# Three edits to a fused recurrent attention, low-rank mixing and gated FFN kernel: the order of the first loads, the slots of three mixing tiles, the order of the attention output products

## The reference: a recurrent state, then two dense layers

```
f = sigmoid(f_logit)
for t in tokens:   state = f[t, :, None] * state + outer(k[t], v[t]);   y[t] = q[t] @ state
x = y as (4, 768, 384)
u = x + (low-rank mixing over tokens: U is 768x32, V is 32x768)
x2 = u + relu(u @ w_ch1) @ w_ch2                       # 384 -> 1536 -> 384
h = relu(x2 @ w_in)                                    # 384 -> 1024
out = (h * sigmoid(conv3 over tokens of h)) @ w_out    # 1024 -> 384
```

## The kernel before, in words

| (par, ch) | quarter in kind 0 | quarter in kind 1 |
|---|---|---|
| (0, 0) | A: rows 0, columns 0 | A |
| (0, 1) | B: rows 0, columns 1 | C |
| (1, 0) | C: rows 1, columns 1 | B |
| (1, 1) | D: rows 1, columns 0 | D |

## Time and profile before

### The profile page before, as it was taken

How to read it: one execution, slowest core, us unless ns; L and a number is a source line. 1 busy time by engine, 2 the same in 40 slices (tenths; PEclk the granted TensorE clock), 3 DMA queues, 4 the chain that set the end, 5 groups by cost and what they waited for, 6 DMA issues and landing times.

```text
span 713.4 us, 22514 instructions
## 1 busy us (share of the span) xinstructions
PE 684.9 (96%) x10076; PEld 648.7 (91%) x10076; DVE 438.8 (62%) x744; ACT 248.8 (35%) x508; POOL 266.1 (37%) x243
## 2 busy tenths in 40 slices
PE   2888999999999999999999999999999999999997
PEld 1788799999999999999999899999999989999997
DVE  6886675674786764364597855365498651122875
ACT  1034534251355412223245432213145541121553
POOL 4872574463542333152263315143263220030432
PEclk9999999999999999999999999999999999999999
DMA  9331444432002111201201110200000100000000
GB/s 207 94 93 37 113 135 118 118 90 62 8 18 74 35 34 25 68 4 28 64 2 56 46 57 3 68 24 25 24 2 2 35 34 1 0 1 1 1 34 33
DMA packets 22719, 33.46 MB, mean 47 GB/s; under 512 B 3584, under 2 KB 15616, under 8 KB 22624
## 3 DMA queue, kind: packets, MB, share of 16 engines
q1 hardware_dynamic: 21616, 30.27, 15.4%
q10 hardware_dynamic: 1008, 1.77, 1.1%
HBM read 27.31 MB, written 4.72 MB: 45 GB/s over the span
## 4 chain that ended last, share of the span: by engine, by line
PE 91%; POOL 2%; DVE 2%; issue 2%; ACT 1%; DMA 1%; ACTq 0%; POOLq 0%; DVEq 0%
PE acc L751 8%; PE att L614 7%; PE hb L732 7%; PE acc L752 7%; PE acc L756 7%; PE hb L733 7%; PE hb L734 7%; PE acc L790 5%; PE hb L771 5%; PE hb L773 5%; PE hb L772 5%; PE acc L791 5%; PE acc L795 5%; PE att L660 3%; PE att L636 1%
## 5 line engine op out<-in xcount | busy, mean ns | idle before, releaser
L1138 DVE SCALAR_TENSOR_TENSOR r_lo<-hb,r_hi 128x386 fp32r<-128x386 f32 (+1 forms) x96 | 53.5, 557 | 179.1 <-ACT r_hi L914 179.1
L914 ACT ACTIVATE r_hi<-hb 128x386 fp32r<-128x386 f32 (+1 forms) x96 | 47.2, 491 | 248.8 <-PE hb L734 248.8
L1227 POOL TENSOR_TENSOR k_t<-k_t,blocks 112x512 f32<-112x512 f32 x60 | 81.2, 1356 | 135.0 <-PE att L614 127.2
L1266 POOL TENSOR_TENSOR r_lo<-conv,r_hi 128x384 fp32r<-128x384 f32 x64 | 63.3, 989 | 141.6 <-ACT r_hi L929 141.6
L751 PE MATMUL acc<-r_hi,w_ch_hi 128*128 128x386 f32 (+1 forms) x288 | 103.1, 358 | 0.0
L732 PE MATMUL hb<-u_hi,w_ch_hi 128*128 128x386 f32 (+1 forms) x288 | 98.1, 341 | 1.2 <-POOL w_ch_lo L1239 0.7
L733 PE MATMUL hb<-u_hi,w_ch_lo 128*128 128x386 f32 (+1 forms) x288 | 97.5, 339 | 0.0
L752 PE MATMUL acc<-r_hi,w_ch_lo 128*128 128x386 f32 (+1 forms) x288 | 97.3, 338 | 0.0
L734 PE MATMUL hb<-u_lo,w_ch_hi 128*128 128x386 f32 (+1 forms) x288 | 96.9, 336 | 0.0
L1168 DVE SCALAR_TENSOR_TENSOR conv<-hb,convw,conv 128x384 f32<-128x384 f32 x128 | 79.1, 618 | 4.5
L614 PEld LDWEIGHTS att<-q_t,k_t 48*64 48x64 f32 (+3 forms) x3840 | 59.3, 134 | 19.0 <-issue 13.2
(11 more groups left out here) (147 smaller groups left out, 1258.0 us busy)
## 6 DMA issues: line engine op xcount, KB each, us to landing
v_p<-in_vn_dram SPq DMA_DIRECT2D x12, 384.0 KB, 3.7
out_dram<-ostage SPq DMA_DIRECT2D x24, 192.0 KB, 2.1
q_t<-in_qT_dram SPq DMA_DIRECT2D x21, 192.0 KB, 3.5
k_t<-in_kT_dram SPq DMA_DIRECT2D x21, 192.0 KB, 3.4
gates<-in_fT_dram SPq DMA_DIRECT2D x21, 192.0 KB, 3.6
ostage<-in_w_ch_dram SPq DMA_DIRECT2D x14, 192.0 KB, 2.6
conv<-in_w_ch_dram SPq DMA_DIRECT2D x10, 192.0 KB, 3.0
ostage<-in_w_out_dram SPq DMA_DIRECT2D x5, 192.0 KB, 2.4
```

## The change

In words: (1) Loads of duos 0 to 2 go in the order gates, q, k on both queues; mask and identity are issued behind duo 0's loads. (2) GpSimd clears gates ahead of k, and takes over two of the three score buffers after that. (3) VectorE prepares identity and masks after gating q of duo 0, no longer ahead of the selves. (4) For duo 0 alone VectorE gates the even k itself, ahead of the even q, with a semaphore of its own (`k_first_ready`); GpSimd makes the gate-pair products of duo 0 as soon as the sigmoid is done. (5) Mixing tiles 3, 4 and 5 follow slots 0, 1 and 2. (6) The 64 output products of a duo are issued in another order, with the wait on `carried` behind 32 of them.

```diff
             if s < 2 * N1:
                 order.append(("first1", b, s))
-                if s < 2:
-                    order += [("mix", b, CT + i) for i in ([0], [1, 2])[s]]
+                if s < CT:
+                    order.append(("mix", b, CT + s))
...
-            consts()
             for task in ORDER:
...
+                    load_f(n)
                     load_q(n)
                     load_k(n)
-                    load_f(n)
+                    if n == 0:
+                        consts()
...
-                    pe.wait_ge(k_ready, gated(n, max(st - 1, 0)))
+                    k_gated(pe, n, max(st - 1, 0))
...
+                    for u in range(2):
+                        for r in range(PAIRS):
+                            add(0, u, r, 0, 0)
+                            add(0, u, r, 0, 1)
+                            mm = add(0, u, r, 1, 0)
+                    mm.then_inc(carried, 1)
+                    for r in range(PAIRS):
+                        add(0, 0, r, 1, 1)
+                        add(1, 0, r, 0, 0)
+                    pe.wait_ge(carried, outputs(n))
+                    for u in range(2):
+                        for r in range(PAIRS):
+                            add(1, u, r, 0, 1)
+                            add(1, u, r, 1, 0)
+                            add(u, 1 - u, r, 1, 1)
+                            mm = add(1, 1, r, u, u)
                     mm.then_inc(y_done, 1)
...
-            for i in range(3):
-                nc.vector.memset(scores[i][:], 0.0).then_inc(cleared_s, 1)
+            nc.vector.memset(scores[0][:], 0.0).then_inc(cleared_q, 1)
...
                     dve.wait_ge(gates_ready, n + 1)
                     dve.wait_ge(selves_ready, selves(n))
+                    if n == 0:
+                        nc.vector.tensor_tensor(even_k, even_k, split_blocks(gates[i][0:PR, :], 1)[:, :, 1, 0],
+                                                ALU.mult).then_inc(k_first_ready, 1)
                     nc.vector.tensor_tensor(even, even, split_blocks(gates[i][0:PR, :], 1)[:, :, 0, 0],
                                             ALU.mult).then_inc(q_ready, 1)
+                    if n == 0:
+                        constants()
...
             for i in range(3):
+                nc.gpsimd.memset(gates[i][32:64, :], 0.0).then_inc(cleared_k, 1)
                 nc.gpsimd.memset(k_t[i][32:64, :], 0.0).then_inc(cleared_k, 1)
-                nc.gpsimd.memset(gates[i][32:64, :], 0.0).then_inc(cleared_k, 1)
             pool.wait_ge(cleared_k, 6)
+            for i in range(1, 3):
+                nc.gpsimd.memset(scores[i][:], 0.0).then_inc(cleared_s, 1)
...
-                if st == 0:
+                if (n, st) == (0, 0):
+                    pool.wait_ge(gates_ready, 1)
+                elif st == 0:
```

More of the change, by code:

```diff
@@ L178 @@
 LAST_AT = numbered(lambda t: t[0] == "att" and t[2] == LEVELS - 1)
[L179 removed]
+GATED_AT = numbered(lambda t: t[0] == "att" and t[2] < LEVELS and t[2] != 0 and t[1:] != (0, EVEN))
 PAIRED_AT = numbered(lambda t: t[0] == "att" and t[2] in (EVEN, 1))
@@ L438, in products_made, with k_gated @@
                 engine.wait_ge(merged_ready, merged(n, st - 1))
+        def k_gated(engine, n, st):
+            if st == 0 and n == 0:
+                engine.wait_ge(k_first_ready, 1)
+            else:
+                engine.wait_ge(k_ready, gated(n, st))
         def weights_split(engine, n):
@@ L643, in attention @@
                     begun = set()
[L644 to L663, removed]
-                        if kind == 0:
-                            mm.then_inc(carried, 1)
-                            pe.wait_ge(carried, outputs(n))
@@ new lines, in add @@
+                    def add(kind, u, r, par, ch):
+                        cc, g, o = 2 * u + ch, u * PAIRS + r, C * (par ^ ch)
+                        gg = par * 2 * PAIRS + g
+                        if kind == 0 and j == 0 and cc == 0:
+                            return None
+                        if kind == 0:
+                            rows, first = slice(C * par, C * par + D), at(u, r, ch)
+                            lhsT = q[rows, first:first + C]
+                            rhs = state[rows, (4 * j + cc) % STATES, r, :]
+                        else:
+                            rows = slice(C * ch, C * ch + C)
+                            lhsT = scores[i][rows, gg * C:(gg + 1) * C]
+                            rhs = v_p[i][rows, 2 * g + par, :]
+                        start = (par, ch) not in begun
+                        begun.add((par, ch))
+                        return pe.matmul(banks[o:o + C, par, g * D:(g + 1) * D], lhsT, rhs, start=start,
+                                         stop=(kind == 1), skip_group_check=True)
@@ L823, in load @@
                     act.wait_ge(q_ready, scaled(0, EVEN))
+                act.wait_ge(cleared_k, 2 * n + 1)
+                act.dma_start(gates[n][odd, :].rearrange("d (u t) -> d u t", u=2),
+                              fT[0, 2 * n:2 * n + 2, 1].rearrange("u d t -> d u t")).then_inc(loaded_f[n], 16)
                 act.wait_ge(cleared_q, n + 1)
@@ L991, in _, with constants @@
                     nc.vector.memset(part[:, :, col:col + PAD].bitcast(F32), 0.0).then_inc(padded, 1)
[L992 to L1002, removed]
+            def constants():
+                dve.wait_ge(loaded_masks, 32)
+                nc.vector.tensor_copy(ident_r[:], x[:, 1, 0:P]).then_inc(padded, 1)
+                nc.vector.tensor_copy(masks[:].rearrange("p l t -> p (l t)"), x[:, 0, 0:LEVELS * 32]).then_inc(masks_ready, 1)
+                pair, odd = x[:, 0, 0:32], x[:, 0, 256:288]
+                units = x[:, 1, 0:P].rearrange("p (h n two) -> p h n two", h=2, two=2)
+                first = first_mask[:].rearrange("p (n two) -> p n two", two=2)
+                nc.vector.tensor_copy(first[:, :, 0], pair).then_inc(masks_ready, 1)
+                nc.vector.tensor_tensor(odd, units[:, 0, :, 1], units[:, 1, :, 1], ALU.add).then_inc(masks_ready, 1)
+                dve.wait_ge(masks_ready, 3)
+                nc.vector.tensor_tensor(first[:, :, 1], odd, pair, ALU.add).then_inc(masks_ready, 1)
             def take_scores(n, st):
@@ L1221, in attention @@
                     pool.wait_ge(level_done, levels(n, st))
-                    pool.wait_ge(k_ready, gated(n, st - 1))
+                    k_gated(pool, n, st - 1)
                     products_made(pool, n, st)
```

19 lines of the change are left out of this document (10 added, 9 removed).

## The result

The changed kernel has a median of 716.88 us (17 runs, 715.34 to 718.53), the kernel before 715.43 us in the same comparison (17 runs). The ratio is 1.0023, 95% interval 1.0013 to 1.0033: slower by 1.6 us (0.9 to 2.4). Forecast were 718.6 us and slower; the range, 715.2 to 721.6, holds it, but the likeliest case's size, +3.5, is more than twice the measured one. The profiled execution of after took 717.44 us, its span 715.6, 2.2 more than before.

The account below looks back on a forecast made before the run. TensorE, busy 96% of the span, was taken to bound the kernel. Terms -1.9 - 1.4 + 4.1 + 2.7 = +3.5 us on the profiled 715.21 gave 718.7, forecast as 718.6 us; 8-in-10 range 715.2 to 721.6.

Parts of the forecast that it names:

- start: Loads and gating of duo 0: level 0 starts near 11.35 instead of 13.21, -1.9 us (ends -2.4 and -1.2).
- mixing slots: First-FFN groups behind tile 5, batches 1 to 3: three waits on VectorE go, -1.4 us (ends -1.6 and 0).
- products, duos 3 to 11: Dense output products: quarter D ends last, 2.56 us instead of 2.10, nine times +0.46, +4.1 us (ends +3.6 and +5.8).
- products, duos 0 to 2: Slower output products at 0.106 us a round: 0.9 us each, all in the chain, +2.7 us (ends +1.5 and +3.3).
- the prediction's own borders: Whole kernel: faster below 713.0 us (0.14), slower above 717.2 (0.72), the same between (0.14); 0.3% is 2.1 us.
- rival b: Output products: each starts only after all ahead in the program; 48 rounds, 2.73 us, total 721.0 us; chance 0.06.
- The 23 loads: Duo 9's output products: 23 loads started after 0.47 us, in the ninth round; strict order gives at most 20.
- the cover of duo 1: Duo 1's loads: last may land at 14.7, needed at 15.2; if late, takes back at most some 0.5 us.
- the prediction's own signs of being wrong: Output group under 2.1 us, time below 715, or duo 1's selves waiting for k would show the forecast wrong.
- I carry the whole gain forward: From level 0 on each step is released by the one before, so the start's whole -1.9 us was kept.
- The prediction's 1.62 / 15: Duos 0 to 2: (1.84 - 0.22) / 15, given as 0.106 us a round of output products.
- rival (d): Duos 0 to 2: cost hidden behind ScalarE's copies and state updates, 58 to 76 us; 715.9 us, no change; chance 0.07.

Follow-up runs that it names:

- start alone: The kernel before with parts 1 to 4 of the change only (loads, clearings, constants, k of duo 0 on VectorE): 715.12 us, ratio 0.9989.
- constants first: The kernel before with the change's start, but the DMAs of masks and identity issued ahead of duo 0's gates, as before: 712.89 us, ratio 0.9947.
- 32 rounds behind the wait: The kernel before with the change's product order, but the four middle D products also behind the wait: 729.34 us, ratio 1.0189.
- balanced order alone: The kernel before with all kind 0 products, eight of kind 1 in A and D, the wait, then B and C: 714.06 us, ratio 0.9977.
- mixing slots with the balanced order: The kernel before with the change's mixing slots and the product order of balanced order alone: 712.85 us, ratio 0.9947.
- all three parts: The changed kernel with the masks' and identity's DMAs first and the product order of balanced order alone: 710.24 us over 4 runs, ratio 0.9904.

## Why the prediction was right and where it was wrong

| term | forecast | measured |
|---|---|---|
| start | -1.9 (-2.4 to -1.2) | -0.8 (-1.6 to +0.1), alone; 0.3 of it at the end of the span |
| mixing slots | -1.4 | -1.33 (three of 0.44 to 0.45) |
| products, duos 3 to 11 | +4.1 | +4.05 (nine of 0.45) |
| products, duos 0 to 2 | +2.7 | -0.4 (-1.2 to +0.4), alone |
| sum | +3.5 | +1.5; the change itself +1.6 |

The direction rests on the dense products, and they were right. The size is out by two misses of opposite sign: the start gave 1.1 us less than forecast, and duos 0 to 2 cost 3.1 us less. That they cancel in part is luck. Had the start given its forecast 1.9 us, the change would have cost 0.4 us, next to nothing. By the prediction's own borders (faster below 713.0, slower above 717.2) the measured 716.88 counts as the same, to which it gave 0.14; the interval of the ratio still leaves out no change.

**Products in the dense stages: right, mechanism and size.** A quarter takes one load in 58 ns whatever the others do, and the group ends when the fullest quarter does. Three orders with 16, 24 and 32 rounds of the fullest quarter behind the wait take 2.30, 2.75 and 3.22 us. That also settles strict order (rival b): it wanted 0.63 a duo (nine of them 5.7, where the prediction's upper end has 5.8). By the Trainium skill's page "TensorE: Matmul & The Clock Gate", section "Part 3: Packing small matmuls", matmuls of different tiles start strictly in program order; the 0.45 a duo disagree. The 23 loads that the prediction held against it are weight loads, which the same section lets overlap with matmuls in flight; the matmul records decide. In duo 4 they start over 2.17 us before and 2.61 after: 0.44 more, and not 0.63. So what the section on the chip says of each engine, that it takes its instructions "in the order in which they were written", does not hold on TensorE from one quarter to another.

**Mixing: right.** No wait of a first-FFN group on VectorE is left behind a tile, and slot by slot 0.44 us are gone.

**Start: right as far as level 0, wrong behind it.** Level 0 came at 10.90, forecast 11.35. The sentence that failed is the cover of duo 1: its last load "may land at 14.7"; in after its selves wait for k until 15.77, and with the start alone until 16.81, since the DMA rate drops to 183 and 170 GB/s. That duo 1's selves wait for k was one of the prediction's own signs of being wrong, and it came. I had allowed "at most some 0.5 us"; at level 2 of duo 0 1.0 of the 2.3 us are gone, since GpSimd gates duo 1's k first (17.34 to 19.22) and has duo 0's, which level 2 waits for, queued behind it. In these two profiles 0.9 more are gone at T of duo 0, and 0.6 of them in one place: TensorE stands still, with no releaser, in front of level 5's last products. Timeline of PE before, then of after, then of the start with the constants first:

```profile
42.28 0.26 PE L614 MATMUL acc<-q_t,k_t 48*48 48x32 f32 x1
43.05 1.50 PE L614 MATMUL acc<-q_t,k_t 48*48 48x32 f32 x63 [0.50 <-issue]
```
```profile
41.26 0.26 PE L623 MATMUL acc<-q_t,k_t 48*48 48x32 f32 x1
42.61 1.50 PE L623 MATMUL acc<-q_t,k_t 48*48 48x32 f32 x63 [1.09 <-issue]
```
```profile
41.15 0.26 PE L622 MATMUL acc<-q_t,k_t 48*48 48x32 f32 x1
43.32 1.50 PE L622 MATMUL acc<-q_t,k_t 48*48 48x32 f32 x63 [1.92 <-issue]
```

The stop lies behind the same record in each; in the three profiles of the unchanged program it lasts 0.50, 0.90 and 1.37 us. One pair of profiles says little about it, so here are means, of nine profiles with the old start, of the three with the change's start, and of the two with the constants first:

| | old start | change's start | constants first |
|---|---|---|---|
| level 0 of duo 0 | 13.39 | 11.14 (-2.25) | 11.82 (-1.57) |
| level 2 of duo 0 | 23.06 | 22.09 (-0.97) | 21.45 (-1.61) |
| T of duo 0 | 45.24 | 44.49 (-0.75) | 44.26 (-0.98) |

So with the change's start 1.3 us go at the late k of duo 1 and 0.2 up to T; with the constants first none go there, and 0.6 up to T. "I carry the whole gain forward" was the wrong step. The -0.8 at T and the 0.3 at the end of the span together lie within the ratio's -1.6 to +0.1.

**Products of duos 0 to 2: the term that decided the miss.** Where TensorE stays slow, the price is the forecast one: from Y of duo 0 to the next T it is 4.86 us with the new order, 3.89 in the undisturbed old one (start alone), +0.97 for 0.9; and the kernel with 32 rounds behind the wait pays 5.5 us for a worked-out 5.1. (The prediction's 1.62 / 15 is 0.108; the 0.106 follows when the 20 ns between the first and the fourth quarter of a round are left out.) In duos 1 and 2 together the change cost only 0.36 (T of duo 2 to rank: 11.97 and 11.61). What is wrong is the premise that the slow pace of the earlier trace rows holds up to the rank products. In the first profile it does, in the second one of the same program it doesn't; PEld there, duos 1 and 2 (against the earlier trace rows):

```profile
64.75 1.05 PEld L660 LDWEIGHTS acc<-state,q_t 48*64 48x64 f32 x64
66.01 0.90 PEld L660 LDWEIGHTS acc<-v_p,scores 64*64 64x64 f32 x52 [0.20 <-PE acc L660]
67.60 0.25 PEld L660 LDWEIGHTS acc<-v_p,scores 64*64 64x64 f32 x10 [0.69 <-issue]
...
69.05 0.89 PEld L660 LDWEIGHTS hb<-v_p,scores 64*64 64x64 f32 x51 [0.21 <-PE hb L660]
71.15 0.31 PEld L660 LDWEIGHTS hb<-v_p,scores 64*64 64x64 f32 x13 [1.21 <-issue]
```

The slow pace goes with TensorE's clock at half, where the prediction read a granted 1.00: the first point of the last section has the rows. At the fast pace the array runs into stops of the "issue" kind. In after both meet in duo 2 (timeline of PEld):

```profile
70.84 0.89 PEld L670 LDWEIGHTS hb<-state,q_t 48*64 48x64 f32 x43
...
72.35 0.56 PEld L670 LDWEIGHTS hb<-v_p,scores 64*64 64x64 f32 x22
74.07 0.54 PEld L670 LDWEIGHTS hb<-v_p,scores 64*64 64x64 f32 x13 [1.17 <-issue]
```

The group is fast, then stops for 1.17 us, and its end comes 0.36 us behind the slow one of before. So rival (d), 715.9, was nearer in this term, though by another road: not hidden behind ScalarE, but absorbed by a clock that rises in the middle and by stops. That the price is absorbed in the median is shown by three comparisons, -0.4 (order in duos 0 to 2), -0.1 (order alone) and -0.2 (the change less start and mixing); how, is read from single profiles. What makes the clock rise at 70 us in after and at 75 before is not settled.

**Left open.** By the ratios five kernels win more than their edits' steps add up to (their ratio, less the dense part and the third slot, less 0.8 for a new start): mixing slots alone 1.5 us, balanced order alone 1.5, constants first 3.0, mixing slots with the balanced order 2.3, all three parts 4.6. Up to 1.1 us of the last three may be the reference, which ran at 716.44 there while its unchanged twin took 715.35. In four of the five profiles the pace rises between 58 and 61 us, with the mixing slots alone at 64; in the first profile of the kernel before it does at 75. The early part goes with that moment in the main:

| program | pace rises at | early |
|---|---|---|
| unchanged, three profiles | 63.2; 75.2; 77.2 | 104.01; 106.81; 108.19 |
| all three parts; balanced order | 58.1; 59.5 | 103.70; 104.05 |
| constants first; mixing and balanced order | 59.9; 60.5 | 104.91; 105.76 |
| change; order alone | 70.3; 70.3 | 106.70; 107.71 |
| start alone | 75.0 | 106.19 |
| 32 rounds behind the wait | 87.6 | 113.45 |
| pace falls back later: start and mixing; order in duos 0 to 2; mixing slots alone | 59.4; 62.6; 64.2 | 106.08; 107.09; 106.89 |

Whether the edits bring the early rise about, or the layout of the program, or chance, no run tells apart: each kernel but the unchanged one has one profile.

## What to carry to other kernels

On a packed array count the rounds of each quarter on either side of a wait, not the products: the fullest quarter behind the wait sets the end, and filling a drain helps only in the quarters that are idle in it. Before a gain at the start is carried forward, ask for each later load what now stands ahead of it in its queue, and for each shared engine whose work it takes first. And take a second profile of the same program: it shows which stretch repeats (here to 0.03 us in 464) and which moves by itself (here 4 us in 107), before any row of the second is given a price. Where one shape of load has two lengths, look for the clock first, and don't take a printed 1.00 for a record.

## What the runs showed of the hardware

- **The slow pace goes with the half clock, and the column hides it.** A float32 load with 64 columns takes 223 ns or 135, and four quarters start one each in 106 or 58 ns. The clock's column reads 1.00 for the slow stretch of the unchanged program, yet the traces have no record of the clock there: in all 14 the first record, at 1.00, starts where the pace rises (75.19 us in the first profile, 63.24 and 77.18 in the other two of this program), and what lies ahead of it is printed as 1.00. In three kernels the pace falls back later, where there are records, and they say 0.50, the lower of the two levels (1.2 and 2.4 GHz): mixing slots alone, 71.05 to 77.88 us; new order in duos 0 to 2, 66.04 to 69.45; start and mixing, 79.91 to 83.32. In the first two of these stretches the loads of 64 columns take 223 ns again. That the slow pace ahead of the first record is the half clock too is read from these equal lengths; no record shows it. Stretches of the kernel with the mixing slots alone (columns as in the earlier trace rows, the clock third from the end):

```profile
65.00:70.00 5.00, 3.56 (x224) 3.32 (x227) 3.07 (x7) 2.39 (x6) 0.48 (x1) 1.00 0.26 48
71.00:77.50 6.50, 5.39 (x84) 2.90 (x80) 1.11 (x3) 1.24 (x3) 3.89 (x5) 0.50 0.47 121
78.00:82.00 4.00, 3.09 (x74) 2.53 (x67) 2.01 (x6) 3.29 (x8) 1.81 (x2) 1.00 0.15 32
```

  The first rise comes between 58 and 77 us, and at 88 in the kernel with 32 rounds behind the wait. Before the rise at 75 TensorE was busy for 3.91 of the 4 us from 68 to 72; it had been busy for 4.00 of 4 us from 56 to 60, and no rise followed for 15 us. In the 7 us before each fall TensorE's longest idle stretch was 1.29, 1.48 and 0.89 us. The Trainium skill's page "TensorE: Matmul & The Clock Gate", section "Part 1: The HAM clock gate (the "warmup" mystery)", gives 106.7 and 55.6 ns between starts of 128 columns at 1.2 and 2.4 GHz. If a float32 record makes two passes of 64 columns (an estimate that no run tests), the measured 106 and 58 agree. The page also has the moment of the change vary by 500 ns from run to run; here it varies by 14 us between executions of one program.
- **Stops of TensorE without a releaser**, 0.5 to 1.9 us, at the same record in different executions, in the first 75 us only. Single packets of the queue named "instruction" lie near them; that they are the cause is not shown.
- **DMA share and rate part.** From 8 to 11 us the transfers moved 183 GB/s at a share of 1.11 with the constants in the middle of one queue, and 228 and 255 at 1.06 with them first.
